# One combining addition in the run products, a negated copy from ScalarE, and the mask ahead of them

## The chip, the cores and the metric

One core of one Trainium2 chip. The metric is the device time of one execution of the whole program in microseconds (us); lower is better. Engines: TensorE (PE), VectorE (DVE), ScalarE (ACT), GpSimd (POOL) and SyncE (SP), which issues the DMAs.

## The reference

Three stages, all in fp32. First a linear recurrence with a complex decay for each channel, for 4 x 8 heads, 768 tokens and 48 channels:

```python
mag = np.sqrt(a_re * a_re + a_im * a_im)
scale = np.minimum(mag, 0.999) / (mag + 1e-06)
a_re_n, a_im_n = a_re * scale, a_im * scale
for t in range(S):
    new_re = ar * S_re - ai * S_im          # ar, ai: row t of a_re_n, a_im_n
    new_im = ar * S_im + ai * S_re
    S_re, S_im = new_re + k[t] * v[t], new_im   # outer product
    y[t] = q[t] @ S_re
```

Then `softplus(x @ w_in) @ w_out` over the 3072 tokens (384 to 2048 to 384), and then `((x @ w1) * (x @ w2)) @ w3 @ w_out` (384 to 1024 to 384).

## The kernel before

The recurrence is turned into masked attention. With p the product of all normalised `a` from the start of the sequence on (a complex number for each token and channel), q is multiplied by p and k divided by it; then y = mask(q' k'^T) v plus a carried state. The products p are made by a scan on VectorE, over tiles of 384 tokens with channels on the partitions (3 groups of 128 channels, 1152 elements in each of the two parts):

- Tokens are laid out in runs of 8 (`RUN`), so that element i of all runs lies together: 144 elements for each part. `prep_run(i)`, i = 1 to 7, multiplies element i of every run by the product up to i-1. One such complex product (`cmul`, L870) is two products of 288 elements into `ms` (L872, L873: `a` by the real part and by the imaginary part), a drain, then two combining instructions of 144 elements (L875: real, a difference; L876: imaginary, a sum), and a drain.
- `prep_carry` scans over the run ends (the same `cmul` on `gp`), `prep_by` applies the carries, `prep_p_` combines, `prep_q_` and `prep_keys` scale q and k.
- Ahead of the runs, ScalarE and VectorE normalise `a`: squares, logarithm, exponential, a Newton step, and last `prep_a` (L905), which multiplies both parts of `an` in place.

There are 8 tiles (m = 0 to 7). Tiles 0 and 1 are prepared in a prologue, together with the rounding of the weights into a high and a low part (`raw_high` on ScalarE, `raw_low` on VectorE). Then come 8 slots (n = 0 to 7). Slot n does the softplus layer for tile n in 8 steps (j = 0 to 7), the attention products of tile n+1 in its first six, and (n = 0 to 5) the preparation of tile n+2. Slots 1 to 4 are in a loop of two rounds on each engine; slots 0 and 5 to 7 are written out, so that their waits have constants. The order is written by hand for each engine:

- TensorE (`slot`, L1337) for each j: the up product of j+1, the scores of j, the down product of j, the outputs of j. The up product of j+1 has to wait until VectorE has added the relu of step j (`add_relu`, L1114, the **sum** below; semaphore p_sum), because that frees PSUM. The outputs wait for the mask (`mask_scores`, L1066, semaphore a_masked).
- ScalarE (L760) for each j: softplus of j+1 (absolute value L696, the k copy L682, exponential L700, logarithm L702), then the rounding `g_high` (L709), which waits for the sum.
- VectorE (L1129) for each j: the pieces of preparation `before_mask[j]`, the mask, `after_mask[j]`, the sum, `after_sum[j]`, then `g_low` (L1121). The three tables are at L1026 to L1029. In j = 0 that is: `a`, run step 1, mask, run step 2, sum, run step 3, `g_low`.

A stage for the last layer follows (6 tiles of 512 tokens), with no preparation in it. `tt` is the buffer that takes the scaled q, which SyncE stores to DRAM (`store_q`, semaphore q_wr).

Of the kernel before, what the change touches and what calls it, by code (L numbers as in the profile page):

```python
# [8 lines left out]
ALU = mybir.AluOpType  # L9
ACT = mybir.ActivationFunctionType  # L10
# [6 lines left out]
P = 128  # L17
# [5 lines left out]
GT = G * T  # L23
# [19 lines left out]
def build(nc, a_re, a_im, q, k, v, w_in, w_out, w1, w2, w3t, w_out2, qk_scr, y_scr, x2_scr, w34_scr, out):  # L43
    with ExitStack() as ctx:
        def sem(name):
            return ctx.enter_context(nc.semaphore(name))
# [5 lines left out]
        def sb(name, shape, dt=F32, at=None):  # L52
            size = 4
            for n in shape[1:]:
                size *= n
            if at is None:
                at = Map.at
                Map.at += -(-size // 32) * 32
            return nc.alloc_sbuf_tensor_at(name, shape, dt, offset=at), at
# [15 lines left out]
        x1l, _ = sb("x1l", [P, G, T], F32R)  # L75

        x1raw, _ = sb("x1raw", [P, G, T])
        an, at_att = sb("an", [P, 2, GT])
        qk, _ = sb("qk", [P, 2, GT])
        pp, _ = sb("pp", [P, 2, GT])  # L80
        tt, _ = sb("tt", [P, 2, GT])
        te, _ = sb("te", [P, 2, GT])
        tr, _ = sb("tr", [P, GT])
        stq, _ = sb("stq", [P, H, T])
# [82 lines left out]
        prep_sq = sem("prep_sq")  # L167
        prep_m2 = sem("prep_m2")
        prep_rs = sem("prep_rs")
        prep_p = sem("prep_p")  # L170
        prep_psq = sem("prep_psq")
        prep_p2 = sem("prep_p2")
# [451 lines left out]
        def _(eng):  # L624
# [5 lines left out]
            def raw_high(i):  # L630

                eng.wait_ge(raw_ld[RAW[i]], 16 * RAW[:i + 1].count(RAW[i]))
                act(piece_to[i][0], piece(i), ACT.Copy).then_inc(raw_hi, 1)
# [17 lines left out]
            def prep_rsqrt(m, first=False):  # L651
# [4 lines left out]
                    eng.wait_ge(prep_k, m)  # L656
                act(tr[:, :], te[:, 1, :], ACT.Square).then_inc(prep_rs, 1)

            def prep_psquares(m):
                eng.wait_ge(prep_p, m + 1)  # L660
                act(te[:, 0, :], pp[:, 0, :], ACT.Square)
                act(te[:, 1, :], pp[:, 1, :], ACT.Square).then_inc(prep_psq, 1)
# [17 lines left out]
            def k_by_tokens(m, i):  # L680
                eng.wait_ge(a_mm, NG * m + i + 1)
                act(kt[:, i % 2, :, :], ps_kt, ACT.Copy).then_inc(kt_ev, 1)  # L682
# [7 lines left out]
            def softplus(n, j, split, between=None):  # L690

                eng.wait_ge(g_lo, after(n, j))
                for us in parts(split):
                    buf = sp[:, j % 2, us, :]
                    eng.wait_ge(p_mm, after(n, j, us))
                    act(buf, ps_u[j][:, us, 0:T], ACT.Abs)  # L696
                    if between is not None:
                        between()
                    eng.drain()
                    act(buf, buf, ACT.Exp, scale=-1.0)  # L700
                    eng.drain()
                    act(buf, buf, ACT.Ln, bias=1.0).then_inc(sp_log, us.stop - us.start)  # L702

            def g_high(n, j, split):

                eng.wait_ge(g_free, (NP1 - 1) * n + max(j, 1))
                for us in parts(split):
                    eng.wait_ge(p_sum, after(n, j, us) + 2)
                    act(g_h[:, j % GR, us, :], sp[:, j % 2, us, :], ACT.Copy).then_inc(g_hi, us.stop - us.start)  # L709
# [3 lines left out]
            prep_log(0)  # L713
            prep_rsqrt(0, first=True)
            raw_high(1)
            raw_high(2)
            raw_high(3)
            prep_psquares(0)
# [3 lines left out]
            prep_rsqrt(1)  # L722
            for mi in range(NM2):
                w34_rows(mi)
            for i in range(4, 7):
                raw_high(i)
            k_by_tokens(0, 0)
            for i in range(NG):
                if i + 1 < NG:
# [30 lines left out]
            def slot(n, att, has_prep, nxt_prep, nxt=True, weights=False):  # L760
                split = not att
                for j in range(NP1):
                    if att and 1 <= j <= NG:
                        y_out(n + 1, j - 1)
                    if has_prep and j == 4:
                        prep_psquares(n + 2)
                    if has_prep and j == 5:
                        prep_inverse(n + 2)
                    if nxt_prep and j == 6:
                        prep_squares(n + 3)  # L770
                    if j < NP1 - 2:
                        softplus(n, j + 1, split, (lambda: k_by_tokens(n + 1, j)) if att else None)
                        g_high(n, j + 1, split)
                    elif j == NP1 - 2:

                        def next_x1():
                            y_loaded(n + 1)
                            x1_high(n + 1)

                        softplus(n, j + 1, split, next_x1 if nxt else None)  # L780
                        if nxt_prep:
                            prep_log(n + 3)
                        g_high(n, j + 1, split)
                        if nxt_prep:
                            prep_rsqrt(n + 3)
                    elif nxt:
                        softplus(n + 1, 0, False)
                        g_high(n + 1, 0, False)
                    if weights and j < 2 * G:
                        w2_high(j)  # L790
                    elif weights and j == 2 * G:
                        w34_high()

                if nxt:
                    eng.wait_ge(x1_lo, n + 2)
                x2_out(n)
# [60 lines left out]
        def _(eng):  # L857
# [7 lines left out]


            runs = an[:, :, :].rearrange("p c (a i r) -> p c a i r", i=RUN, r=CR)
            carries = gp[:, :, :].rearrange("p c (g r) -> p c g r", g=G)

            def cmul(out_r, out_i, a, br, bi, m1, m2):  # L870

                ve.tensor_tensor(m1, a, br, ALU.mult)  # L872
                ve.tensor_tensor(m2, a, bi, ALU.mult)  # L873
                eng.drain()  # L874
                ve.tensor_tensor(out_r, m1[:, 0], m2[:, 1], ALU.subtract)  # L875
                ve.tensor_tensor(out_i, m1[:, 1], m2[:, 0], ALU.add)  # L876
                eng.drain()
# [25 lines left out]

            def prep_a(m):
                ve.scalar_tensor_tensor(out=an[:, :, :], in0=an[:, :, :], scalar=-1e-6,  # L905
                                        in1=tr[:, :].unsqueeze(1).to_broadcast([P, 2, GT]), op0=ALU.mult, op1=ALU.mult)
                eng.drain()

            def prep_run(i):

                cmul(runs[:, 0, :, i, :], runs[:, 1, :, i, :], runs[:, :, :, i - 1, :],
                     runs[:, 0:1, :, i, :].to_broadcast([P, 2, GC, CR]), runs[:, 1:2, :, i, :].to_broadcast([P, 2, GC, CR]),
                     ms[:, 0:2 * GC * CR].rearrange("p (c a r) -> p c a r", c=2, a=GC),
                     ms[:, 2 * GC * CR:4 * GC * CR].rearrange("p (c a r) -> p c a r", c=2, a=GC))

            def prep_carry_start(even):
                if even:
# [72 lines left out]
            def prep(m, even, pieces, first=False):  # L990

                for piece in pieces:
                    if piece == "m2":
                        prep_m2_(m)
                    elif piece == "newton":
                        prep_newton(m)
                    elif piece == "scale":
                        prep_scale(m)
                    elif piece == "a":
                        prep_a(m)  # L1000
                    elif piece == "ends":
                        prep_carry_start(even)
                    elif piece == "p":
                        prep_p_(m, even, first)
                    elif piece == "q":
                        prep_q_(m)
                    elif piece == "p2":
                        prep_p2_(m)
                    elif piece == "inverse":
                        prep_inv_newton(m)  # L1010
                    elif piece == "keys":
                        prep_keys(m)
                    elif piece[0] == "run":
                        prep_run(piece[1])
                    elif piece[0] == "carry":
                        prep_carry(piece[1])
                    else:
                        prep_by(m, piece[1], piece[2], first)

            def steps(name, *which):  # L1020
                return [(name, s_) for s_ in which]
# [1 line left out]
            by = [("by", c, part) for part in range(2) for c in range(2)]  # L1023


            before_mask = {0: ["a"] + steps("run", 1), 1: steps("run", 4, 5), 2: ["ends"] + steps("carry", 1, 2), 3: by[:2],  # L1026
                           4: ["q"], 5: ["inverse"]}
            after_mask = {0: steps("run", 2), 1: steps("run", 6), 2: steps("carry", 4, 8), 3: by[2:], 4: [], 5: []}
            after_sum = {0: steps("run", 3), 1: steps("run", 7), 2: steps("carry", 16, 32), 3: ["p"], 4: ["p2"], 5: ["keys"]}  # L1029

            def raw_low(i):
# [438 lines left out]
```

## Time and profile before

| | |
|---|---|
| median of 3 executions | 1051.46 us (1050.67 to 1052.08) |
| the profiled execution | 1052.62 us |
| its span, first to last instruction | 1050.8 us |
| TensorE matmul busy | 933.9 us (89%) |
| VectorE busy | 613.4 us (58%), 997 instructions |
| ScalarE busy | 426.8 us (41%), 602 instructions |
| mean granted TensorE clock | 0.953 of full speed |

The profile is one execution recorded by the hardware. In its listings a row has the start in us from the span's start, the duration, the engine, the line of the kernel, the operation with output and inputs, and in brackets how long the engine had been idle before it and which instruction released it. "issue" means that the engine waited for nothing that the profile shows. PEclk is the clock granted to TensorE as a share of full speed.

### The profile page before, as it was taken

What the parts mean: (1) busy time and instruction counts of PE and PEld (TensorE: products, weight loads), DVE (VectorE), ACT (ScalarE), POOL (GpSimd) and SP (SyncE); (2) the same over time, 40 slices, a digit from 0 to 9 for tenths busy, and PEclk for the clock granted to TensorE, in tenths of its full rate; (3) what the DMA queues carried; (4) which work ended last, traced back from release to release, by engine and by line L of the source; (5) the groups of instructions that cost most, each with busy time, mean ns of one, the idle gap of its engine ahead of it and who ended that gap; (6) DMA issues with size and microseconds to landing.
All of it is one profiled execution on the core that took longest, in us unless ns stands there. A gap on an engine that the chain in (4) does not pass through costs nothing.

```text
span 1050.8 us, 15307 instructions
## 1 busy us (share of the span) xinstructions
PE 933.9 (89%) x5538; PEld 841.2 (80%) x5538; DVE 613.4 (58%) x997; ACT 426.8 (41%) x602; POOL 70.2 (7%) x56
## 2 busy tenths in 40 slices
PE   0965659989989989989989999999899999999998
PEld 0544559988979979879879899899788888888887
DVE  5977878878879879879888732345221212121211
ACT  3161253663664664654654654478011111111011
POOL 0000000000000000000000000000121212121311
PEclk9985569999999999999989999999899999999999
DMA  9584183480470560560660440042101010101000
GB/s 337 205 219 146 44 197 80 132 198 12 137 192 13 144 184 13 147 182 11 172 160 8 136 107 12 9 166 79 44 1 60 1 60 0 60 0 60 1 31 31
DMA packets 99382, 99.54 MB, mean 95 GB/s; under 512 B 7664, under 2 KB 92656, under 8 KB 99312
## 3 DMA queue, kind: packets, MB, share of 16 engines
q1 hardware_dynamic: 99312, 98.60, 32.8%
q8 instruction: 45, 0.74, 0.3%
q14 instruction: 25, 0.20, 0.1%
HBM read 63.96 MB, written 29.88 MB: 89 GB/s over the span
## 4 chain that ended last, share of the span: by engine, by line
PE 52%; DVE 22%; DVEq 9%; ACT 7%; issue 5%; DMA 3%; SPq 2%; ACTq 0%
PE ps_p L1222 6%; PE ps_p L1223 6%; PE ps_p L1224 6%; DVE sp L1114 3%; PE ps L1222 3%; PE ps L1224 3%; PE ps L1223 3%; DVEq L874 3%; PE ps_ay L1258 3%; PE ps L1404 3%; PE ps L1406 2%; PE ps L1405 2%; DVE ms L872 2%; SPq L404 2%; DVE g_l L1121 2%
## 5 line engine op out<-in xcount | busy, mean ns | idle before, releaser
L1222 PE MATMUL ps<-g_h,wo_h 128*128 128x384 f32 x384 | 134.9, 351 | 6.0 <-DVE g_l L1121 5.3
L615 POOL TENSOR_TENSOR abl<-ab,abh 128x512 fp32r<-128x512 f32 x48 | 69.3, 1444 | 972.2 <-DVE abh L1204 972.2
L1224 PE MATMUL ps<-g_h,wo_l 128*128 128x384 f32 x384 | 129.7, 338 | 0.0
L1223 PE MATMUL ps<-g_l,wo_h 128*128 128x384 f32 x384 | 129.5, 337 | 0.0
L1222 PE MATMUL ps_p<-x1h,win_h 128*128 128x384 f32 x336 | 119.1, 354 | 9.1 <-DVE sp L1114 7.0
L1224 PE MATMUL ps_p<-x1h,win_l 128*128 128x384 f32 x336 | 114.8, 342 | 0.0
L1223 PE MATMUL ps_p<-x1l,win_h 128*128 128x384 f32 x336 | 114.7, 341 | 0.0
L709 ACT ACTIVATE g_h<-sp 128x768 fp32r<-128x768 f32 (+1 forms) x71 | 55.4, 781 | 109.2 <-DVE sp L1114 108.7
L1258 PE MATMUL ps_ay<-stq,stk 96*128 96x128 f32 x384 | 58.4, 300 | 38.7 <-DMA vt<-in_v 12.7
L1195 DVE TENSOR_TENSOR ab<-ps_ay,bc 128x512 f32<-128x512 f32 x24 | 16.6, 693 | 123.8 <-ACT bc L841 123.8
L1258 PEld LDWEIGHTS ps_ay<-stq,stk 96*128 96x128 f32 x384 | 54.3, 212 | 43.0 <-issue 30.2
L1222 PEld LDWEIGHTS ps<-g_h,wo_h 128*128 128x128 f32 x384 | 72.9, 190 | 11.0 <-DVE g_l L1121 9.6
L696 ACT ACTIVATE sp<-ps_p 128x768 f32<-128x768 f32 (+1 forms) x63 | 46.4, 737 | 86.4 <-PE ps_p L1224 86.4
L1114 DVE SCALAR_TENSOR_TENSOR sp<-ps_p,sp 128x768 f32<-128x768 f32 (+1 forms) x63 | 54.6, 867 | 45.7 <-ACT sp L702 42.4
L1195 DVE TENSOR_TENSOR ab<-ps_p,bc 128x512 f32<-128x512 f32 x24 | 16.6, 692 | 110.6 <-ACT bc L841 110.6
L1121 DVE TENSOR_TENSOR g_l<-sp,g_h 128x768 fp32r<-128x768 f32 (+1 forms) x71 | 62.3, 878 | 22.0 <-ACT g_h L709 16.2
L1222 PEld LDWEIGHTS ps_p<-x1h,win_h 128*128 128x128 f32 x336 | 65.0, 194 | 11.4 <-DVE sp L1114 8.3
L1223 PEld LDWEIGHTS ps<-g_l,wo_h 128*128 128x128 f32 x384 | 73.0, 190 | 0.0
L1224 PEld LDWEIGHTS ps<-g_h,wo_l 128*128 128x128 f32 x384 | 72.7, 189 | 0.0
L841 ACT ACTIVATE bc<-ps_p 128x512 f32<-128x512 f32 x24 | 14.4, 599 | 136.4 <-PE ps_p L1224 136.4
L841 ACT ACTIVATE bc<-ps_k 128x512 f32<-128x512 f32 x24 | 14.4, 599 | 125.2 <-PE ps_k L1224 125.2
L1223 PEld LDWEIGHTS ps_p<-x1l,win_h 128*128 128x128 f32 x336 | 65.1, 194 | 0.0
(149 smaller groups left out, 2082.9 us busy)
## 6 DMA issues: line engine op xcount, KB each, us to landing
qk_scr<-tt SPq DMA_DIRECT2D x16, 576.0 KB, 5.5
stq<-qk_scr SPq DMA_DIRECT2D x48, 192.0 KB, 4.6
qk_scr<-pp SPq DMA_DIRECT2D x16, 576.0 KB, 4.0
stk<-qk_scr SPq DMA_DIRECT2D x48, 192.0 KB, 4.6
an<-in_a_re SPq DMA_DIRECT2D x8, 576.0 KB, 4.2
an<-in_a_im SPq DMA_DIRECT2D x8, 576.0 KB, 5.2
qk<-in_q SPq DMA_DIRECT2D x8, 576.0 KB, 8.2
qk<-in_k SPq DMA_DIRECT2D x8, 576.0 KB, 9.2
```

What stands on the lines that cost most here:

```text
L615: tensor_tensor(abl[:, m % AR, :], ab[:, m % 2, :], abh[:, m % AR, :].bitcast(F32), ALU.subtract).then_inc(ab_lo, 1)
L696: act(buf, ps_u[j][:, us, 0:T], ACT.Abs)
L709: act(g_h[:, j % GR, us, :], sp[:, j % 2, us, :], ACT.Copy).then_inc(g_hi, us.stop - us.start)
L874: eng.drain()
L1114: ve.scalar_tensor_tensor(out=buf, in0=ps_u[j][:, us, 0:T], scalar=0.0, in1=buf, op0=ALU.max, op1=ALU.add)\
L1121: ve.tensor_tensor(g_l[:, j % GR, us, :], sp[:, j % 2, us, :], g_h[:, j % GR, us, :].bitcast(F32), ALU.subtract).then_inc(g_lo, us.stop - ...
L1195: ve.tensor_tensor(ab[:, m % 2, :], ps_ab[m % 2][0], bc[:, m % 2, :], ALU.mult).then_inc(ab_mul, 1)
L1222: mm(o, wh, xh, start=start, stop=False)
L1223: mm(o, wh, xl, start=False, stop=False)
L1224: return mm(o, wl, xh, start=False, stop=stop)
L1258: mm(ps_a[:, h4, :], stk[0:D2, h, cs], stq[0:D2, h, cs], start=True, stop=True)
L1404: mm(ps_o[s_], ah, w34h[:, m, :], start=m == 0, stop=False)
```

## The change

The two combining instructions of a run step become one of 288 elements. For it the second product is formed with the pair (imaginary part, minus imaginary part), and its halves are read in exchanged order: real = m1[0] + m2[1], imaginary = m1[1] + m2[0]. The negated imaginary part is made by ScalarE into `tt[:, 0]`, which is free at that time; `an` and `tt` become neighbours in one tensor `at4`, so that a view `runs_n` takes in the imaginary part and its negative. ScalarE waits for `prep_a` (new semaphore prep_an) and, but for the first tile, for the store of the tile before out of `tt`; VectorE waits for ScalarE ahead of run step 1 (new semaphore prep_neg). In the slots run step 1 goes from ahead of the mask to behind it. `prep_carry` keeps `cmul`.

```diff
-        an, at_att = sb("an", [P, 2, GT])
+        at4, at_att = sb("at4", [P, 4, GT])
+        an, tt = at4[:, 0:2, :], at4[:, 2:4, :]
...
-        tt, _ = sb("tt", [P, 2, GT])
...
+            def prep_negate(m, first=False):
+                eng.wait_ge(prep_an, m + 1)
+
+                if not first:
+                    eng.wait_ge(q_wr, 32 * m)
+                act(tt[:, 0, :], an[:, 1, :], ACT.Copy, scale=-1.0).then_inc(prep_neg, 1)
...
             prep_rsqrt(0, first=True)
             raw_high(1)
+            prep_negate(0, first=True)
             raw_high(2)
...
                 w34_rows(mi)
-            for i in range(4, 7):
-                raw_high(i)
+            raw_high(4)
+            prep_negate(1)
+            raw_high(5)
+            raw_high(6)
...
                         softplus(n, j + 1, split, (lambda: k_by_tokens(n + 1, j)) if att else None)
+                        if has_prep and j == 0:
+                            prep_negate(n + 2)
                         g_high(n, j + 1, split)
...
+            runs_n = at4[:, 1:3, :].rearrange("p c (a i r) -> p c a i r", i=RUN, r=CR)
...
             def prep_a(m):
                 ve.scalar_tensor_tensor(out=an[:, :, :], in0=an[:, :, :], scalar=-1e-6,
-                                        in1=tr[:, :].unsqueeze(1).to_broadcast([P, 2, GT]), op0=ALU.mult, op1=ALU.mult)
-                eng.drain()
-
-            def prep_run(i):
-
-                cmul(runs[:, 0, :, i, :], runs[:, 1, :, i, :], runs[:, :, :, i - 1, :],
-                     runs[:, 0:1, :, i, :].to_broadcast([P, 2, GC, CR]), runs[:, 1:2, :, i, :].to_broadcast([P, 2, GC, CR]),
-                     ms[:, 0:2 * GC * CR].rearrange("p (c a r) -> p c a r", c=2, a=GC),
-                     ms[:, 2 * GC * CR:4 * GC * CR].rearrange("p (c a r) -> p c a r", c=2, a=GC))
+                                        in1=tr[:, :].unsqueeze(1).to_broadcast([P, 2, GT]), op0=ALU.mult, op1=ALU.mult)\
+                    .then_inc(prep_an, 1)
+                eng.drain()
+
+            def prep_run(m, i):
+
+                if i == 1:
+                    eng.wait_ge(prep_neg, m + 1)
+                m1 = ms[:, 0:2 * GC * CR].rearrange("p (c a r) -> p c a r", c=2, a=GC)
+                m2 = ms[:, 2 * GC * CR:4 * GC * CR].rearrange("p (c a r) -> p c a r", c=2, a=GC)
+                ve.tensor_tensor(m1, runs[:, :, :, i - 1, :], runs[:, 0:1, :, i, :].to_broadcast([P, 2, GC, CR]), ALU.mult)
+                ve.tensor_tensor(m2, runs[:, :, :, i - 1, :], runs_n[:, :, :, i, :], ALU.mult)
+                eng.drain()
+                ve.tensor_tensor(runs[:, :, :, i, :], m1, m2[:, ::-1, :, :], ALU.add)
+                eng.drain()
...
-            before_mask = {0: ["a"] + steps("run", 1), 1: steps("run", 4, 5), 2: ["ends"] + steps("carry", 1, 2), 3: by[:2],
+            before_mask = {0: ["a"], 1: steps("run", 4, 5), 2: ["ends"] + steps("carry", 1, 2), 3: by[:2],
                            4: ["q"], 5: ["inverse"]}
-            after_mask = {0: steps("run", 2), 1: steps("run", 6), 2: steps("carry", 4, 8), 3: by[2:], 4: [], 5: []}
+            after_mask = {0: steps("run", 1, 2), 1: steps("run", 6), 2: steps("carry", 4, 8), 3: by[2:], 4: [], 5: []}
```

## Rows read from the trace of the kernel before

**Rows 1.** The page's chain that ended last, shares of the span by engine.
```profile
PE 52%; DVE 22%; DVEq 9%; ACT 7%; issue 5%; DMA 3%; SPq 2%; ACTq 0%
```

**Rows 2.** VectorE, slot n=2: start us, us, what [idle us <-releaser].
```profile
307.75 2.55 DVE L905 SCALAR_TENSOR_TENSOR an<-an,tr 128x2304 f32<-128x2304 f32 x1
310.37 0.46 DVE L872 TENSOR_TENSOR ms<-an 128x288 f32<-128x288 f32 x1
...
311.96 0.69 DVE L1066 TENSOR_TENSOR am<-ps_ay,mask 128x512 f32<-128x512 f32 x1 [0.16 <-issue]
...
314.22 0.96 DVE L1114 SCALAR_TENSOR_TENSOR sp<-ps_p,sp 128x768 f32<-128x768 f32 x1 [0.23 <-issue]
...
323.13 0.96 DVE L1114 SCALAR_TENSOR_TENSOR sp<-ps_p,sp 128x768 f32<-128x768 f32 x1 [0.23 <-issue]
```

**Rows 3.** ScalarE in the same slot, same columns: its last work before the sum.
```profile
308.78 0.85 ACT L702 ACTIVATE sp<-sp 128x768 f32<-128x768 f32 x1
```

**Rows 4.** TensorE, same slot: waits for mask and sum.
```profile
312.71 0.43 PE L1281 MATMUL ps_ay<-stq,state 96*48 96x128 f32 x4 [1.43 <-DVE am L1066]
...
315.23 0.45 PE L1222 MATMUL ps_p<-x1h,win_h 128*128 128x384 f32 x1 [0.63 <-DVE sp L1114]
```

**Rows 5.** VectorE in the prologue, tile m=0: normalisation and the first run step.
```profile
19.26 2.56 DVE L905 SCALAR_TENSOR_TENSOR an<-an,tr 128x2304 f32<-128x2304 f32 x1
21.90 0.46 DVE L872 TENSOR_TENSOR ms<-an 128x288 f32<-128x288 f32 x1
...
22.80 0.31 DVE L875 TENSOR_TENSOR an<-ms 128x144 f32<-128x144 f32 x1
23.03 0.30 DVE L876 TENSOR_TENSOR an<-ms 128x144 f32<-128x144 f32 x1
23.40 0.46 DVE L872 TENSOR_TENSOR ms<-an 128x288 f32<-128x288 f32 x1
```

**Rows 6.** Groups by form on VectorE: count, busy us, mean ns, idle before.
```profile
L872 DVE TENSOR_TENSOR ms<-an 128x288 f32<-128x288 f32 x56 | 25.3, 452 | 1.9 <-issue 0.5
```

**Rows 7.** Groups by form on ScalarE: an operation of the negation's size.
```profile
L657 ACT ACTIVATE tr<-te 128x1152 f32<-128x1152 f32 x8 | 9.3, 1166 | 0.5
```

**Rows 8.** ScalarE in the prologue, tile m=0.
```profile
31.53 1.48 ACT L633 ACTIVATE win_h<-raw 128x1536 fp32r<-128x1536 f32 x1 [16.14 <-DMA raw<-in_w_in]
```

**Rows 9.** TensorE in the prologue, tile m=1.
```profile
92.15 2.08 PE L1258 MATMUL ps_ay<-stq,stk 96*128 96x128 f32 x8 [12.43 <-DVE am L1066]
```

**Rows 10.** ScalarE in slot n=0.
```profile
156.60 0.84 ACT L702 ACTIVATE sp<-sp 128x768 f32<-128x768 f32 x1
```

**Rows 11.** VectorE in slot n=0: first and second sum.
```profile
159.33 0.96 DVE L1114 SCALAR_TENSOR_TENSOR sp<-ps_p,sp 128x768 f32<-128x768 f32 x1
...
168.90 0.96 DVE L1114 SCALAR_TENSOR_TENSOR sp<-ps_p,sp 128x768 f32<-128x768 f32 x1 [0.41 <-ACT sp L702]
```

**Rows 12.** ScalarE in slot n=3.
```profile
387.85 0.85 ACT L702 ACTIVATE sp<-sp 128x768 f32<-128x768 f32 x1
```

**Rows 13.** VectorE in slot n=3: first sum.
```profile
391.47 0.96 DVE L1114 SCALAR_TENSOR_TENSOR sp<-ps_p,sp 128x768 f32<-128x768 f32 x1 [0.26 <-issue]
```

**Rows 14.** TensorE, slot n=3: waits for mask and sum.
```profile
389.92 0.65 PE L1284 MATMUL ps_ay<-am,vt 128*48 128x128 f32 x8 [0.42 <-DVE am L1066]
...
392.48 0.44 PE L1222 MATMUL ps_p<-x1h,win_h 128*128 128x384 f32 x1 [1.11 <-DVE sp L1114]
```

**Rows 15.** TensorE, slot n=1: waits for mask and sum.
```profile
235.18 0.64 PE L1284 MATMUL ps_ay<-am,vt 128*48 128x128 f32 x8 [1.44 <-DVE am L1066]
...
237.75 0.69 PE L1222 MATMUL ps_p<-x1h,win_h 128*128 128x384 f32 x1 [1.11 <-DVE sp L1114]
```

**Rows 16.** VectorE in slot n=5: first and second sum.
```profile
544.80 0.96 DVE L1114 SCALAR_TENSOR_TENSOR sp<-ps_p,sp 128x768 f32<-128x768 f32 x1
...
555.61 0.96 DVE L1114 SCALAR_TENSOR_TENSOR sp<-ps_p,sp 128x768 f32<-128x768 f32 x1 [0.41 <-ACT sp L702]
```

**Rows 17.** Windows, slot n=5: PE, PEld, DVE, ACT, POOL; then PEclk, DMA.
```profile
547.00:548.00 1.00, 1.00 (x5) 1.00 (x4) 0.86 (x2) 0.00 (x0) 0.00 (x0) 0.50 0.00 0
```

More of the change, by code:

```diff
@@ L169, in build @@
         prep_rs = sem("prep_rs")
+        prep_an = sem("prep_an")
+        prep_neg = sem("prep_neg")
         prep_p = sem("prep_p")
@@ L1013, in prep @@
                     elif piece[0] == "run":
-                        prep_run(piece[1])
+                        prep_run(m, piece[1])
                     elif piece[0] == "carry":
```

## The prediction

> **What bounds the kernel now.** I read the page's chain first: TensorE has half of it, but VectorE and its drains have 31% [rows 1]. So a change on VectorE counts only where the chain runs over VectorE. The listing of the chain in order of time and the timelines show where. In each of the six slots that prepare a tile (n=0 to 5) VectorE works almost without a gap from the normalisation of `a` to the end of j=3; then TensorE takes over. In the prologue both tiles' preparations lie on the chain.
>
> The start of slot n=2 is the pattern. `a` is normalised from 307.75 to 310.30, run step 1 starts at 310.37, the mask at 311.96, the first sum (softplus plus relu) at 314.22, the second at 323.13 [rows 2]. ScalarE ended its logarithm at 309.63 and then only waits for the sum [rows 3]. TensorE waits 1.43 for the mask, computes the outputs, and waits 0.63 more, for the sum, which frees its PSUM banks [rows 4]. The sum, not the mask, is what ends last there.
>
> **Part 1: one addition for two.** A run step takes 1.50 from start to start (21.90 to 23.40). Its two combining instructions last 0.31 and 0.30, but the second starts 0.23 after the first, so together they take 0.60 of those 1.50, from 22.80 to the next step's start [rows 5]. One instruction of 288 elements lasts 0.45, as the product of that size does [rows 6]. With the 0.08 that now lies between the last addition's end (23.33) and the next step it takes 0.53. A step saves 0.07 and takes 1.43. Bounds: nothing, if the addition with its halves exchanged is slower than the product, to 0.15, if instructions did not overlap (0.31 + 0.30 - 0.46). I take 0.07, read from starts. The product with the negated copy has the form of the one it replaces: no cost.
>
> The Trainium skill says otherwise ("VectorE: DVE Perf Modes", The DRAIN you can't avoid): the next instruction starts only when the pipe of the one before is empty. By that a step would save 0.15. The starts above disagree: the second addition begins before the first one ends. The Trainium skill's "Vector Engine (DVE) Microarchitecture Reference" (Measured stream behaviour on trn2) has about 75 ns per instruction left after overlap, and this trace agrees with its 0.07.
>
> **Part 2: the negation and its wait.** A ScalarE pass over 128x1152 takes 1.17 [rows 7]. It starts when `a` is done, or when ScalarE is free if that is later. For each handover I take 0.05, the time from the sum's end (314.22 + 0.96) to TensorE's start [rows 2, 4]. Inside the loop a wait whose value is in a register costs up to 0.16 [rows 2]; ScalarE gets a second such wait, so I add 0.16 there. ScalarE's wait for the store of tt costs nothing: that store was issued in the middle of the slot before, and half a slot of matrix products hides it; if it did not, whatever is left of it would be added to ScalarE's start one for one. On ScalarE the k copy and both functions of softplus are ahead of the negation, and the rounding behind it waits for the sum anyway. Behind the waiting VectorE stand run steps 1 and 2, the sum, and through the sum TensorE.
>
> *Tile 0 in the prologue.* `a` ends at 21.82; step 1 starts at 21.82 + 0.05 + 1.17 + 0.05 = 23.09 in place of 21.90, +1.19 [rows 5]. ScalarE is free: it idles 16.14 before 31.53 [rows 8]. Seven steps return 0.49. **+0.70.**
>
> *Tile 1.* The same +1.19; four steps (0.28) lie ahead of the first mask, which TensorE awaits for 12.43 [rows 9]. Behind that TensorE sets the pace, so steps 5 to 7 return nothing. ScalarE rounds raw pieces 5 and 6 and copies k later, behind the negation; VectorE has step 1, the rest of piece 4 and step 2 ahead of piece 5, and TensorE waits for the mask, not for k; hidden. **+0.91.**
>
> *Slots n=2 and 4.* ScalarE starts at 310.30 + 0.05 + 0.16 and ends at 311.68. The mask, now ahead (about 310.45 to 311.15), fits in that wait and costs nothing. Step 1 starts at 311.73, the sum 2 x 1.43 + 0.16 later at 314.75: +0.53. Steps 3 to 7 return 0.35. **+0.18 each.** So the saving in steps and the mask's free place do not quite pay for the wait.
>
> *Slot n=0.* ScalarE is late here: its logarithm ends at 157.44 [rows 10]. Step 1 at 158.66, first sum at 161.52 in place of 159.33. Before the change VectorE had slack: the second sum waited for ScalarE [rows 11]. Its own pace from sum to sum is 8.91 in slot 2 [rows 2], less 0.28 for four steps (3 to 6) and about 0.3 for register waits which this unrolled slot lacks: second sum at 169.85 in place of 168.90, and step 7 returns 0.07. **+0.9.**
>
> *Slots n=1 and 5.* In slot 5 the granted clock fell to half (1.2 GHz) [rows 17], in slot 1 too: its first product behind the wait shows 0.69, against 0.45 in slot 2 [rows 15, 4]. The second sum waits for ScalarE, which waits for TensorE: from sum to sum 10.81, not 8.91 [rows 16, 2]. The delay of 0.53 goes through and only step 7 returns anything. **+0.46 each.**
>
> *Slot n=3.* Again ScalarE is late, its logarithm ending at 388.70 [rows 12]; sum at 388.70 + 1.17 + 0.05 + 3.02 = 392.94 in place of 391.47 [rows 13]: +1.47. Five steps would return 0.35, giving +1.12. But see part 3.
>
> **Part 3: what becomes late next.** With the mask ahead, TensorE goes from the down product straight to the outputs, and all its idle time comes behind them in one piece, longer by the sum's delay. In slot 3 it idled 0.42 + 1.11 = 1.53 [rows 14]; that becomes 3.00. In slot 1 it idled 1.44 + 1.11 = 2.55 and the clock fell [rows 15]; in slot 2 it idled 2.06 and it did not [rows 4]. So I expect one more fall, and put it at slot 3. Its price is 10.81 - 8.91 = 1.90 [rows 16, 2], and steps 3 to 6 return nothing. **Slot 3: +1.47 + 1.90 - 0.07 = +3.30.** Slots 2 and 4 come to 2.59 and may fall too; that is a rival. The bounds for the clock as a whole are -3.8 (both falls gone) and +6 (three more).
>
> **Sum.** 0.70 + 0.91 + 0.9 + 2 x 0.18 + 2 x 0.46 + 3.30 = +7.1. Behind slot 5 nothing changes. The profiled execution lasted 1052.62 (span 1050.80 and 1.82 around it); it would become 1059.7. The median shown is 1.16 lower: 1051.46 + 7.1 = **1058.6**.
>
> **Rivals.**
> - *The clock falls no oftener.* Slot 3 costs 1.12, the sum is +4.9: 1056.4. For it: in slots 2 and 3 it has held so far.
> - *It falls in slots 2 and 4 as well*: 2 x (1.90 + 0.28) more, 1063. For it: 2.59 of idle is as much as slot 1 had.
> - *It falls nowhere*, since the mask no longer holds TensorE back: 4.9 - 3.8 = +1.1, 1052.6. Against it: each idle time grows.
> - *VectorE pays each instruction in full*, 0.15 for a step: 29 of the 56 saved steps count above (7, 4, 5, 1, 5, 1, 5, 1), so 2.3 less, 1056.3. The overlapping starts speak against it. By the rule of the Trainium skill on the drain this would be the outcome.
> - *The merge does not happen*: the exchanged halves make the addition as slow as two. 29 x 0.07 = 2.0 more, 1060.6.
> - *Faster: TensorE is held by the mask.* The mask comes 1.5 earlier (310.45, not 311.96). If the outputs, and not the sum, set when the next up product starts, each of six slots gains up to that: 1.6 (prologue) - 9.0 = -7.4, 1044. It decides only where the sum is ready before the outputs end; it comes 0.63 to 1.11 behind them now [rows 4, 14, 15] and will come later still.
>
> **Chances.** Forecast 0.43, no further fall 0.22, more falls 0.13, no falls 0.08, full price 0.04, no merge 0.05, held by the mask 0.05. About 0.2%, 2.1 us, is what a measurement can tell from no change: 1049.4 to 1053.6. Faster 0.05; within, 0.12 (no falls, and the low edges of the cases at 1056); slower 0.83. The range has to take in 1056.3 to 1060.6 with a microsecond or two for the timings of handovers and instruction reading, most of the step to 1063, and the low side down to where no price of the clock is left: 1053.3 to 1062.
>
> **What would show it.** Right: 56 single additions of 288 elements and about 0.45, run steps 1.43 from start to start; VectorE idle 0.5 to 0.7 for ScalarE ahead of run step 1 in slots 2 and 4, and over 2 in slots 0 and 3; TensorE's wait for the mask gone and its wait for the sum 2.6 to 3; first sums 0.5 later after the normalisation; granted clock at half in three of the slots 1 to 5. Wrong: the wait for the negation absent, the first sum no later than now, a slot's length from `a` to `a` shorter in slots 2 and 4, or steps that save 0.15.

## The result, and the profile after

| | before | changed |
|---|---|---|
| median | 1051.07 us (1048.87 to 1052.08, 4 executions) | 1062.61 us (1061.73 to 1066.2, 4 executions) |
| the profiled execution | 1052.62 us | 1062.17 us |
| its span | 1050.8 us | 1060.4 us |

The ratio is 1.0108, with a 95% interval of 1.0084 to 1.0133: slower by some 11.5 us, where 7.1 was forecast, and 0.6 us above the end of the range. The two profiled executions differ by less, by 9.55.

The page of the changed kernel: VectorE is busy 3 us less and has 56 instructions fewer; ScalarE has 8 more.

```profile
PE 933.4 (88%) x5538; PEld 840.7 (79%) x5538; DVE 610.3 (58%) x941; ACT 436.0 (41%) x610; POOL 70.3 (7%) x56
...
PE 51%; DVE 23%; ACT 8%; DVEq 8%; issue 5%; DMA 3%; SPq 2%; ACTq 0%
```

The groups by form on VectorE answer to [rows 6]. There are 56 single additions (L936) of 459 ns, where two instructions of 309 and 302 ns were; L933 and L934 are the two products, and the idle time ahead of L933 is the wait for the negation, L667:

```profile
L936 DVE TENSOR_TENSOR at<-ms 128x288 f32<-128x288 f32 x56 | 25.7, 459 | 4.2
L933 DVE TENSOR_TENSOR ms<-at 128x288 f32<-128x288 f32 x56 | 25.4, 453 | 8.4 <-ACT at L667 6.7 <-issue 0.5
L934 DVE TENSOR_TENSOR ms<-at 128x288 f32<-128x288 f32 x56 | 25.3, 451 | 0.0
```

The start of slot n=2 on VectorE answers to [rows 2]:

```profile
312.90 2.55 DVE L922 SCALAR_TENSOR_TENSOR at<-at,tr 128x2304 f32<-128x2304 f32 x1
315.63 0.69 DVE L1089 TENSOR_TENSOR am<-ps_ay,mask 128x512 f32<-128x512 f32 x1 [0.18 <-issue]
316.69 0.46 DVE L933 TENSOR_TENSOR ms<-at 128x288 f32<-128x288 f32 x1 [0.37 <-ACT at L667]
...
318.12 0.46 DVE L933 TENSOR_TENSOR ms<-at 128x288 f32<-128x288 f32 x1
...
319.72 0.96 DVE L1137 SCALAR_TENSOR_TENSOR sp<-ps_p,sp 128x768 f32<-128x768 f32 x1 [0.23 <-issue]
...
328.36 0.96 DVE L1137 SCALAR_TENSOR_TENSOR sp<-ps_p,sp 128x768 f32<-128x768 f32 x1 [0.24 <-issue]
```

ScalarE's negation started at 315.48, 0.03 behind the end of `a` (315.45):

```profile
315.48 1.17 ACT L667 ACTIVATE at<-at 128x1152 f32<-128x1152 f32 x1 [0.69 <-DVE at L922]
```

`a` starts at 312.90, the mask 2.73 later, run step 1 (316.69) has waited 0.37 for ScalarE behind the mask, and the sum comes 6.82 behind `a` where it came 6.47 behind it. The next run step starts at 318.12, 1.43 behind the first. From the first sum to the second it is 8.64, against 8.91. On TensorE the wait for the mask is gone, and the one for the sum is 2.46 where 1.43 and 0.63 stood [rows 4]:

```profile
320.73 0.45 PE L1245 MATMUL ps_p<-x1h,win_h 128*128 128x384 f32 x1 [2.46 <-DVE sp L1137]
```

In the prologue run step 1 waits 1.23 for ScalarE, where it followed at once [rows 5], and the next step starts 1.44 later:

```profile
19.30 2.56 DVE L922 SCALAR_TENSOR_TENSOR at<-at,tr 128x2304 f32<-128x2304 f32 x1
23.09 0.46 DVE L933 TENSOR_TENSOR ms<-at 128x288 f32<-128x288 f32 x1 [1.23 <-ACT at L667]
...
24.53 0.46 DVE L933 TENSOR_TENSOR ms<-at 128x288 f32<-128x288 f32 x1
```

In slot n=0 ScalarE is late, as the logarithm [rows 10] let expect, and VectorE idles 2.22:

```profile
155.44 2.56 DVE L922 SCALAR_TENSOR_TENSOR at<-at,tr 128x2304 f32<-128x2304 f32 x1
158.10 0.69 DVE L1089 TENSOR_TENSOR am<-ps_ay,mask 128x512 f32<-128x512 f32 x1
161.01 0.46 DVE L933 TENSOR_TENSOR ms<-at 128x288 f32<-128x288 f32 x1 [2.22 <-ACT at L667]
...
163.95 0.96 DVE L1137 SCALAR_TENSOR_TENSOR sp<-ps_p,sp 128x768 f32<-128x768 f32 x1
...
173.62 0.96 DVE L1137 SCALAR_TENSOR_TENSOR sp<-ps_p,sp 128x768 f32<-128x768 f32 x1 [0.48 <-ACT sp L712]
```

And this row has no counterpart before. At the second round of VectorE's loop, slot n=3, the normalisation of `a` waits 3.28 us for nothing that the profile shows:

```profile
389.70 0.96 DVE L1144 TENSOR_TENSOR g_l<-sp,g_h 128x768 fp32r<-128x768 f32 x1
393.94 2.56 DVE L922 SCALAR_TENSOR_TENSOR at<-at,tr 128x2304 f32<-128x2304 f32 x1 [3.28 <-issue]
...
397.81 0.46 DVE L933 TENSOR_TENSOR ms<-at 128x288 f32<-128x288 f32 x1 [0.41 <-ACT at L667]
...
401.26 0.96 DVE L1137 SCALAR_TENSOR_TENSOR sp<-ps_p,sp 128x768 f32<-128x768 f32 x1 [0.65 <-issue]
```

Before, that instruction started at 384.93, 0.88 behind the start of the rounding ahead of it, with no idle time. ScalarE, which the prediction had late in this slot, catches up during the stall: run step 1 waits only 0.41 for it, where over 2 was forecast.

TensorE's clock was at half for a while in four of the slots 0 to 5, where it had been so in two. The windows of TensorE in the changed kernel (its busy time, the granted clock PEclk, DMA share and GB/s) are in slots 0, 1, 3 and 5 and one behind slot 5; a mean of 0.66 over 5 us is 3.4 us at half:

```profile
165.00:170.00 5.00, 5.00 (x21) 0.66 0.32 106
244.00:249.00 5.00, 5.00 (x27) 0.66 0.08 20
397.00:409.00 12.00, 9.12 (x43) 0.57 0.03 9
558.00:563.00 5.00, 4.89 (x19) 0.66 0.07 18
693.00:698.00 5.00, 2.51 (x16) 1.00 0.42 122
```

The same of the kernel before, at the same turns of its slots:

```profile
165.00:170.00 5.00, 5.00 (x40) 1.00 0.06 14
237.00:242.00 5.00, 4.25 (x15) 0.66 0.05 13
392.00:397.00 5.00, 4.52 (x31) 1.00 0.06 15
544.00:553.00 9.00, 8.10 (x41) 0.62 0.06 14
684.00:689.00 5.00, 3.90 (x16) 0.66 0.76 218
```

Stage by stage, from one normalisation of `a` to the next, in the two profiled executions (the rows add up to their difference of 9.55, but for rounding):

| stretch | forecast | profile |
|---|---|---|
| preparation of tile 0 | +0.70 | +0.70 |
| tile 1, up to the first mask | +0.91 | +0.88 |
| rest of the prologue | 0 | +0.79 |
| slot 0 | +0.9 | +1.98 |
| slot 1 | +0.46 | +0.76 |
| slot 2, without the stall | +0.18 | +0.58 |
| the stall, at the turn from slot 2 to 3 | none | +3.28 |
| slot 3 | +3.30 | +2.54 |
| slot 4 | +0.18 | +0.33 |
| slot 5 and all behind it | +0.46 | -2.3 |

The last row is the clock again, at least for the most part: in slot 5 it was at half for 3.4 us where it had been for 6.8 ((1 - 0.62) x 9 / 0.5), and the time from the first sum to the second went from 10.81 to 9.67; and the fall that the kernel before had at 684 did not come.

So is the rest of the prologue. The products behind the last mask came 1.63 later, and by then TensorE's clock was at half: the first of them lasted 0.67 and not 0.42. Before, and then in the changed kernel:

```profile
120.84 0.42 PE L1281 MATMUL ps_ay<-stq,state 96*48 96x128 f32 x4 [1.75 <-DVE state L1075]
```

```profile
122.47 0.67 PE L1304 MATMUL ps_ay<-stq,state 96*48 96x128 f32 x4 [1.26 <-DVE state L1098]
```

### The profile page after: what moved, and what is told of

Same layout as the page of the kernel before. It is cut to its first block, busy times and chain, and to the rows that moved or that the text cites. A ratio compares the mean times of both kernels' runs of the same rounds, so it can differ in the third digit from the quotient of the medians.

```text
span 1060.4 us, 15264 instructions
## 1 busy us (share of the span) xinstructions
PE 933.4 (88%) x5538; PEld 840.7 (79%) x5538; DVE 610.3 (58%) x941; ACT 436.0 (41%) x610; POOL 70.3 (7%) x56
## 4 chain that ended last, share of the span: by engine, by line
PE 51%; DVE 23%; ACT 8%; DVEq 8%; issue 5%; DMA 3%; SPq 2%; ACTq 0%
PE ps_p L1245 6%; PE ps_p L1246 6%; PE ps_p L1247 6%; DVE sp L1137 3%; PE ps_ay L1281 3%; PE ps L1245 3%; PE ps L1247 3%; PE ps L1246 3%; PE ps L1427 3%; PE ps L1429 2%; PE ps L1428 2%; SPq L407 2%; DVE at L936 2%; PE ps_ay L1246 2%; PE ps_ay L1247 2%
```

## Experiments

Three theories stood against each other. **W**: the loss is VectorE's wait for ScalarE, and what the later sum does to TensorE. **R**: part of it is the stall at the loop's second round, which hangs on where VectorE's instructions lie. **C**: the loss is the clock, brought down by idle time in one piece. Each kernel is compared with the kernel before on the same chip.

**e1, the wait without the saving.** In `prep_run`:

```diff
...
-                ve.tensor_tensor(m2, runs[:, :, :, i - 1, :], runs_n[:, :, :, i, :], ALU.mult)
-                eng.drain()
-                ve.tensor_tensor(runs[:, :, :, i, :], m1, m2[:, ::-1, :, :], ALU.add)
...
+                cmul(runs[:, 0, :, i, :], runs[:, 1, :, i, :], runs[:, :, :, i - 1, :],
...
```

The wait for the negation and the mask's place stay as in the changed kernel; the two combining instructions are those of before.

> The changed kernel with the two combining instructions of 144 elements put back; the negation on ScalarE, VectorE's wait for it ahead of run step 1 and the mask ahead of the runs stay (the negated copy is then not read). Theory W (the loss is the wait for ScalarE and what it shifts): no step saves anything, so it is as slow as the changed kernel or slower by up to 29 x 0.07 = 2.0 us: 1062 to 1065; first sums of slots 1, 2, 4 later than before by 0.5 or more behind a's start. Theory R (3.3 us of the loss is one stall of VectorE at the second round of the loop, 3.28 us with no releaser ahead of a's normalisation, which comes with where the shortened program's instructions lie): VectorE has as many instructions again as before, the stall is gone, 1059 to 1061. Theory C (TensorE's clock): the granted clock is at half in slots 0, 1, 3 and 5, as in the changed kernel, and 1062 to 1065.

Measured: 1064.05 us against 1051.84, ratio 1.0132 (1.0093 to 1.0172); its profiled execution took 1060.19. VectorE has no idle time ahead of `a` at the second round. So this kernel is about as slow as the changed one (the intervals overlap) though it has no stall, and the stall goes when the instructions are back. R's 1059 to 1061 was too low, W's 1062 to 1065 holds; the four executions spread from 1060.2 to 1069.2, so nothing finer can be read from the median.

**e2, the saving without the wait.** ScalarE's negation goes out, VectorE does it:

```diff
+                if not first:
+                    eng.wait_ge(q_wr, 32 * m)
+                ve.tensor_scalar(tt[:, 0, :], an[:, 1, :], -1.0, None, ALU.mult)
+                eng.drain()
...
-                    eng.wait_ge(prep_neg, m + 1)
```

> The changed kernel with the negation on VectorE itself, behind a's normalisation (one instruction of 1152 elements, 0.75 us and 0.08 ahead of it, as the scaling of that size), so no wait for ScalarE; merged additions and the mask ahead stay. Theory W: 8 x 0.83 = 6.6 us more work less 0.07 a step (some 41 steps count, 2.9 us) against the kernel before: 1054.8, some 8 below the changed kernel. Theory R: the stall at the loop's second round stays, since the program is as short as the changed one but for one instruction a tile: 1058. Theory C: the clock falls as in the changed kernel, because the idle time of TensorE still lies in one piece behind the outputs: 1057 to 1058.

Measured: 1062.68 us against 1051.84, ratio 1.0101 (1.0071 to 1.0132). The negation takes 760 ns, and tile 0 takes 0.32 more than before (0.83 less 0.49 was expected: 0.34), so the parts are priced right. But the trace stalls 4.3 us at the second round and the clock falls there twice. Against R's 1058 the kernel came out 4.7 higher; only the direction of R is borne out by this run, and where the 4.7 come from stays open.

**e3, the negation hidden.** Steps 1 and 2 keep `cmul`, ScalarE negates elements 3 to 7 only, and the mask is behind run step 1 again:

```diff
+                act(tt[:, 0, :].rearrange("p (a i r) -> p a i r", i=RUN, r=CR)[:, :, 3:, :],
+                    an[:, 1, :].rearrange("p (a i r) -> p a i r", i=RUN, r=CR)[:, :, 3:, :], ACT.Copy, scale=-1.0).then_inc(prep_neg, 1)
...
-                if i == 1:
+                if i < 3:
+                    cmul(runs[:, 0, :, i, :], runs[:, 1, :, i, :], runs[:, :, :, i - 1, :],
...
+                    return
+                if i == 3:
                     eng.wait_ge(prep_neg, m + 1)
```

> Run steps 1 and 2 with the two combining instructions, 3 to 7 merged; ScalarE negates only elements 3 to 7 of the runs (720 of 1152), at the same place, and VectorE waits for it ahead of step 3, behind the first sum; run step 1 is ahead of the mask again. Theory W: the negation ends before the sum in every slot (158.4 against 160.3 in slot 0), nothing waits, and the merged steps return 0.07 each: 1.9 us less than before, less some 0.6 for one more wait on a register: 1049.8. Rival: the merging itself or its semaphores cost something that I have not seen: 1052 or more. Theory R: a stall of about 3.3 at the loop's second round if this program's length hits it too: 1053.

Measured: 1056.4 us against 1051.84, ratio 1.0047 (1.0027 to 1.0067). VectorE waits for no negation, and the trace has the stall, 4.9 us. That is about the whole loss, 4.6; e8 tests it.

**e4, the order alone.** The kernel before with `before_mask[0] = ["a"]` and `after_mask[0] = steps("run", 1, 2)`.

> The kernel before with nothing but run step 1 moved from ahead of the mask to behind it. Theory W: VectorE's order changes but not its work, the first sum comes at the same time, TensorE's wait for the mask goes and its wait for the sum grows by as much: 1051, no change. Theory C: it is the idle time in one piece that brings the clock down (slots 0, 3 besides 1 and 5): 1053 to 1055. Rival (held by the mask): 1047 or less.

Measured: 1052.22 us against 1051.84, ratio 1.0005 (0.9989 to 1.0021): no change. In slot 2 TensorE's idle time is in one piece, 2.11 where it was 1.43 and 0.63:

```profile
315.71 0.44 PE L1222 MATMUL ps_p<-x1h,win_h 128*128 128x384 f32 x1 [2.11 <-DVE sp L1114]
```

Its clock was at half for 3.4 us in slots 1, 2, 4 and 5 (the windows are of slots 2 and 4):

```profile
316.00:321.00 5.00, 5.00 (x23) 0.66 0.08 20
470.00:475.00 5.00, 4.80 (x18) 0.66 0.06 15
```

From the first sum to the second it was 9.67 in slot 2, where 8.91 is the time at full clock: such a short fall costs 0.76, not 1.90, which was the price of the 6.8 us in slot 5. So the clock fell in four slots of this trace, against two in the trace of the kernel before, and the time is the same. Theory C falls as the main cause. That it is the one piece of idle time that brings the clock down is not shown: e11 and e12, below, have the mask behind run step 1, as before, and as many falls.

**e5 and e6, the stall.** e5 is the changed kernel once more. e6 adds 21 drains where VectorE is idle, at 2.4 us; the change took away 21 instructions ahead of the loop (14 in the prologue, 7 in slot 0; its three new waits there are not counted):

```diff
             tokens_mask()
+            for i in range(21):
+                eng.drain()
             prep(0, True, ["m2"])
```

> The changed kernel as it is, for a second trace beside the next one. Theory R: VectorE again stalls about 3.3 us with no releaser at the loop's second round, ahead of a's normalisation, and TensorE's clock falls to half right behind it; 1062. If the stall is chance (not in the trace here), theory R falls.

> The changed kernel with 21 drains on VectorE in its idle time at the very start (2.4 to 9 us): as many instructions as the change took away ahead of the loop, so that the loop's first instruction lies where it lay before. No work added or taken. Theory R: no stall of VectorE at the second round and no 8 KB instruction fetches around 390 us; 3 to 5 us less than the changed kernel: 1058 to 1059. Theory W alone (wait and clock, layout of no matter): 1062, as the changed kernel.

Measured against 1052.34: e5 1065.7 us, ratio 1.0124 (1.0096 to 1.0152); e6 1060.9, ratio 1.0091 (1.0069 to 1.0112). The medians are 4.8 apart, but there are four executions of each, and the two intervals overlap; e3 with e8 and e12, and e7, are the stronger evidence on the time. In the traces the difference is plain. The same instruction in e5 and then in e6:

```profile
390.64 0.96 DVE L1144 TENSOR_TENSOR g_l<-sp,g_h 128x768 fp32r<-128x768 f32 x1
396.60 2.56 DVE L922 SCALAR_TENSOR_TENSOR at<-at,tr 128x2304 f32<-128x2304 f32 x1 [5.00 <-issue]
```

And in e6, with the old start of the loop:

```profile
389.13 0.96 DVE L1146 TENSOR_TENSOR g_l<-sp,g_h 128x768 fp32r<-128x768 f32 x1
390.01 2.55 DVE L922 SCALAR_TENSOR_TENSOR at<-at,tr 128x2304 f32<-128x2304 f32 x1
...
396.24 0.46 DVE L933 TENSOR_TENSOR ms<-at 128x288 f32<-128x288 f32 x1 [2.72 <-ACT at L667]
...
399.30 0.96 DVE L1139 SCALAR_TENSOR_TENSOR sp<-ps_p,sp 128x768 f32<-128x768 f32 x1 [0.27 <-issue]
```

The stall and the wait for ScalarE overlap: with the stall VectorE waits 0.41 for the negation in slot 3, without it 2.72 in e6 and 2.73 in e9, which both have a fall of the clock shortly before, and 0.74 in e1, which has none. From the start of the rounding to the first sum it is 11.56 with the stall of 3.28 and 13.27 with that of 5.00 (e5); without a stall it is 10.17 in e6, 12.13 in e9 and 8.26 in e1. How much of a stall reaches the sum therefore hangs on what else holds up that slot. The clock is part of the price too: in all five traces with the stall TensorE's clock is at half for 6.8 or 10.2 us in slot 3, in the nine without for 3.4 or not at all. The parts were not measured one by one.

Instruction fetches go with the stall. The stretch from 390 to 540 holds most of the second round (393.94 to 550.38 in the first trace of the changed kernel, 390.01 to 548.17 in e6). The queues of the changed kernel in it (packets, MB, share of 16 engines):

```profile
q8 instruction: 9, 0.15, 0.4%
q14 instruction: 5, 0.04, 0.1%
```

Those of e6 in the same stretch, where no line of q14 stands between q8 and the issues:

```profile
q8 instruction: 9, 0.15, 0.4%
issues: line engine op xcount, KB each, median us to landing
```

On q14 the changed kernel fetches 5 times 8 KB, the first of them at the turn; e6, and the kernel before, fetch nothing there on that queue. q8, the other one, serves both alike. The profile does not say which engine q14 serves: that the stall hangs on the place of the loop is shown, that VectorE stands still for want of instructions is concluded from these fetches.

**e7, the stall in the kernel before.** 107 drains, 60 at 2.4 us and 47 at 68.9, in the kernel before.

> The kernel before with 107 drains on VectorE, 60 in the idle time at the start and 47 in the one ahead of the Newton step of tile 1 (68.9 to 72.5 us): with 8 KB fetched at a time (128 instructions of 64 bytes) that is the same shift of the loop as taking 21 away. Theory R: if only the offset within a fetch counts, the kernel before now stalls 3 to 5 us at the loop's second round and takes 1055 to 1057; if the loop's length counts too (it is 14 instructions longer than in the changed one), the stall may be there or not. Theory W alone: 1052, no change.

Measured: 1055.9 us against 1052.34, ratio 1.0035 (1.002 to 1.005). The stall is there, 4.41 us, with the refetches, though no work was added on the chain:

```profile
384.60 0.96 DVE L1126 TENSOR_TENSOR g_l<-sp,g_h 128x768 fp32r<-128x768 f32 x1
389.96 2.56 DVE L905 SCALAR_TENSOR_TENSOR an<-an,tr 128x2304 f32<-128x2304 f32 x1 [4.41 <-issue]
```

Its queue in that stretch:

```profile
q14 instruction: 4, 0.03, 0.1%
```

**e8 and e12, the hidden negation without the stall.** e3 with 15 drains at the start.

> The variant with the negation hidden behind the first sum (steps 3 to 7 merged) and 15 drains on VectorE at the start, as many as the merging took away ahead of the loop. Theory R: the stall of 4.9 us of its trace goes, and the merged steps' 0.07 each are left: 1050 to 1052, at or a little below the kernel before. If it stays at 1056, layout is not the cause.

> The negation hidden behind the first sum, steps 3 to 7 merged, 15 drains: whether it beats the kernel before. By its steps 1.9 us less, by its register wait 0.6 more: a ratio of 0.998 to 1.000. If it is above 1.001, the merging gives nothing here even when nothing waits.

Measured: e8 1052.95 us against 1052.34, ratio 1.0011 (0.9988 to 1.0033); e12 1050.62 against 1051.73, ratio 0.9992 (0.9975 to 1.0008). No stall in either, and of e3's loss 0.6 and -1.1 are left; the merging gives nothing that can be measured, and loses nothing. e12's interval lies wholly below that of e3 (from 1.0027 on); e8's, up to 1.0033, overlaps it a little. A version that beats the kernel before was not found.

**e9, e10, e11, the price of the wait.** e9 is e6 again. e10 and e11 have e6's drains too; e10 doubles ScalarE's part, and e11 puts run step 1 ahead of the mask, and so the mask behind the wait.

The first diff is e10's, the second e11's:

```diff
+                act(tt[:, 1, :], an[:, 1, :], ACT.Copy)
                 act(tt[:, 0, :], an[:, 1, :], ACT.Copy, scale=-1.0).then_inc(prep_neg, 1)
```

```diff
-            before_mask = {0: ["a"], 1: steps("run", 4, 5), 2: ["ends"] + steps("carry", 1, 2), 3: by[:2],
+            before_mask = {0: ["a"] + steps("run", 1), 1: steps("run", 4, 5), 2: ["ends"] + steps("carry", 1, 2), 3: by[:2],
...
-            after_mask = {0: steps("run", 1, 2), 1: steps("run", 6), 2: steps("carry", 4, 8), 3: by[2:], 4: [], 5: []}
+            after_mask = {0: steps("run", 2), 1: steps("run", 6), 2: steps("carry", 4, 8), 3: by[2:], 4: [], 5: []}
```

> The changed kernel with 21 drains at the start, once more, as the base of the next two on the same chip: 1059 to 1062, no stall at the second round.

> The same with a second ScalarE pass of 1152 elements (a plain copy into the other half of tt) ahead of the negation: the wait doubled. Theory W: VectorE waits one pass longer at each of the eight tiles, about 1.1 us each, and the end moves by 8 to 10 us against the base, 1069 to 1071, with TensorE's clock falling in more slots. Rival (the wait is mostly hidden and the loss is the clock): less than 4 us.

> The same base with run step 1 ahead of the mask again, so that VectorE waits for the negation with the mask behind it. Theory W: the mask (0.6 to 0.7) no longer lies in the wait, sums of six slots come 0.6 to 0.8 later, 4 to 5 us more than the base: 1065. Theory C (one piece of idle time brings the clock down): TensorE's idle time is split again and the falls go: 1061 or less.

Measured against 1051.73: e9 1060.56, ratio 1.0078 (1.0054 to 1.0102); e10 1070.42, 1.0173 (1.015 to 1.0197); e11 1064.53, 1.0125 (1.0101 to 1.0149). VectorE's waits for the negation (sum, times, longest) in e9:

```profile
DVE ms L933 <- ACT at L667: 9.1, 8, 2.7
```

In e10, whose lines are one further down:

```profile
DVE ms L934 <- ACT at L668: 17.8, 8, 3.8
```

In e11:

```profile
DVE ms L933 <- ACT at L667: 15.2, 8, 4.0
```

In e10 the wait grows by 8.7 and the time by 9.9. In e11 it grows by 6.1, and the time by 4.0, the 0.6 to 0.7 of a mask in six slots. So a longer wait of VectorE goes into the time nearly whole, and the mask does fit into the wait for free.

e11 also answers theory C, which had 1061 or less because the falls would go. They did not: TensorE's idle time is split again, and its clock is at half for 3.4 us at least once in each of the slots 1 to 5, the same five as in e9. And in e12, with the old order of mask and run step 1, it is so in slots 2, 4 and 5. Slot 2 in e11 and then in e12 (the columns are those of the windows above):

```profile
321.00:326.00 5.00, 4.68 (x19) 0.66 0.06 15
```

```profile
313.00:318.00 5.00, 4.37 (x17) 0.66 0.05 14
```

## Why the forecast was wrong

**The direction, and the mechanism of the wait: right.** The delay of run step 1 in the prologue (23.09 in place of 21.90) and of slot 0's first sum (2.2) came out to 0.05. The first sum of slot 2 came 0.35 later, not 0.53: the negation started 0.03 behind the end of `a`, where I had 0.05 for the handover and 0.16 for a register; ScalarE was idle by then. Without the stall the change costs 8.6 (e6) and 8.8 (e9), where 7.1 was the sum. In e10 the waits of all eight tiles together grow by 8.7 and the time by 9.9, so most of them, if not each, lie on the chain.

**The saving of a step: right.** 1.43 from start to start; 0.07 and not 0.15. The rule of the Trainium skill that the next instruction starts only when the pipe is empty ("VectorE: DVE Perf Modes", The DRAIN you can't avoid) would have had 0.15. The trace disagrees, as it did before. The same section of the Trainium skill has an instruction that is not held start earlier, which the prediction left out; that agrees with the 0.23 between the starts of two additions of 0.31 [rows 5]. The rival of the full price is out, and the one of no merge too.

**The step that failed is part 3, "what becomes late next", and with it the sum.** It looked at engines that wait for each other. The range allowed a microsecond or two for handovers and instruction reading, but no term of the sum was for what 35 instructions fewer in VectorE's program up to the end of the loop (21 ahead of it, 14 in it) do to instruction fetching. In its place the runs showed a stall of 3.28 us at the loop's second round, 5.0 in e5, and a median that is 4.8 lower when the old place of the loop is restored (e6 against e5). e7 shows that it is no matter of the merging: the kernel before stalls as well when its loop is moved, and takes 3.6 us more.

The stall is not simply one more term beside the 7.1. ScalarE's lateness in slot 3, priced at 1.47, is hidden in it (0.41 of waiting where over 2 was forecast), and it comes with a longer fall of the clock. That slot 3 came out near the forecast, +2.54 for 3.30, is therefore partly luck.

**Two terms put at nothing were not nothing.** The rest of the prologue took 0.79 more, and 0.78 to 0.96 more in e5, e6 and e9: each time the last products ran at half clock. "Behind slot 5 nothing changes" was wrong as well: slot 5 and what is behind it took 2.3 less in this trace, and 0.9 to 1.1 less in the other three, where +0.46 was forecast. These two misses work against each other.

**What could have been seen.** Nothing in the trace before could show this stall; a sign that it could be was there, TensorE's own wait of 1.99 us with no releaser at that same turn of the kernel before, which I left out of the argument:

```profile
381.72 0.44 PE L1222 MATMUL ps_p<-x1h,win_h 128*128 128x384 f32 x1 [1.99 <-issue]
```

**The clock: more falls, as forecast; the reason open, and the price too high.** I said one more fall, in slot 3, for 1.90. Two more came in this trace (slots 0 and 3) and in others of this kernel up to five slots have one. But most are of 3.4 us. Such a fall cost 0.76 in e4's slot 2, and in slot 4 of the changed kernel 1.01 (8.65 from sum to sum in the first trace, 9.66 in e5, where the clock fell); slot 3's was of 10.2 us here, behind the stall, and e6 and e9 have two short ones near it. The argument of part 3, that idle time in one longer piece brings the clock down, is not borne out by e11 and e12. The falls differ from execution to execution, in the kernel before too (mean granted clock 0.948 to 0.961 in its executions beside e9), and how much of the 1.5 us between the sum and e6 is theirs stays open.

**Rivals.** *Held by the mask* is refuted by e4, where the mask came 1.5 us earlier and nothing was gained. *No falls* and *no further fall* did not come. *More falls* came in number, at about half the price (0.76 and 1.01 for 1.90).

## What to carry to other kernels

An instruction that is saved on a busy engine is worth its start-to-start time, here 0.07 us, not its duration; one wait for another engine's pass of 1.2 us takes more than seven such steps give back, unless the product of that pass is first needed behind a point where the engine waits anyway (then, in e8 and e12, nothing was lost, and nothing that can be measured was gained). When a program gets shorter or longer ahead of a loop, look at the loop's second round for an idle time without releaser on that engine, and compare with a version padded to the old length before the change is judged.

## What was unexpected

- Taking instructions away can cost time by itself (counted in instructions and drains, without waits). In the five traces of kernels whose VectorE loop starts 15 to 21 instructions earlier than before, or 107 later (the changed kernel, e2, e3, e5 and e7), VectorE stands still 3.3 to 5.0 us at the start of the loop's second round and 8 KB pieces are fetched on q14 again in that round; in the nine others, where the loop starts where it did (the kernel before, e1, e4, e6 and e8 to e12), there is neither. What in the placement decides, and how much code is kept, was not tried.
- The falls of the granted clock in slots 0 to 5 of these traces last 3.4, 6.8 or 10.2 us. A short one cost 0.76 to 1.01 us from sum to sum, the one of 6.8 us 1.90; slots of one and the same order of instructions have them in one trace and not in another.
